# Narrower weight loads in four of six levels of a chunked linear attention

## The chip, the cores and the metric

The kernel runs on one core of one Trainium2 chip. Its time is the device time of one execution in microseconds. Below, TensorE is PE in the profile's rows, its weight loads are PEld, VectorE is DVE, ScalarE is ACT, GpSimd is POOL, and SyncE (which issues most DMAs) is SP.

## The reference, cut to what matters

The program is an attention with a decaying state, then a dense MLP, then a mixture of experts. Only the attention is touched by the change:

```
B, H, S, D = 2, 8, 768, 48
for t in range(S):
    cur = einsum('bhd,bhe->bhde', u * k[t], v[t])
    y[t] = einsum('bhd,bhde->bhe', r[t], state + cur)
    state = w[t][..., None] * state + einsum('bhd,bhe->bhde', k[t], v[t])
x = y.transpose(0, 2, 1, 3).reshape(1536, 384)
```

The MLP computes `relu(x @ w_in)**2 @ w_out` with 2048 hidden columns. The last part picks one of eight experts for each row and applies it.

## The kernel before, in words

**The attention in levels.** The 1536 rows are worked off in six pages of 256 rows (`NG = 6`, index `i`), and a page has two tiles of 128 rows (`t`). A row of a tile belongs to a chunk of 64 (`C = 64`, `h` is the chunk). Inside a chunk, the product of a query (`r`) with an earlier key (`k`) has to carry the decay between the two. The kernel builds this 64x64 matrix per head by doubling. At level `l` the chunk is cut into blocks of `2 * L` rows, with `L = 1 << l`. Keys of the left half of a block meet queries of its right half. TensorE multiplies (`level`, line 600 on), VectorE copies the entries that belong to the level into `AD` by a mask (`select`, line 1206), and VectorE then multiplies decays into keys and queries for the next level (`update`, lines 1192 and 1194). Level `l + 1` of a tile waits for that update (`upd`). There are six levels, 0 to 5.

**One level on TensorE.** The keys are the stationary operand (`x[rows, XW + c:XW + c + n]`, `n` columns), the right halves' 32 queries are the moving operand, and the result has `n` rows in PSUM. The loops over four head pairs, two chunks `h` and two heads `a` make 16 matrix products of 48 x n x 32 for a tile. `a` chooses partitions 0 or 64 for the operands, and `(h + a) % 2` chooses partitions 0 or 64 of PSUM, so four products in a row use the four 64x64 quarters of the array. A product in fp32 is two matmuls, each with its own weight load, in the trace: 32 loads for a tile and level, 64 for both tiles. `n` is `C`, 64, for levels 0 to 4, and 32 for level 5, where ScalarE copies one 32x32 block instead of the masked copy.

The masked copy at level `l` takes, of each pair of blocks, only the keys of the left half. The last left half ends at key `64 - L`. What lies in PSUM behind it isn't taken.

**The order.** Each engine has its own instruction list. A page's levels are not run in one piece. Page `i` is spread over the slots of page `i - 1`'s MLP, which has 16 slots: in a slot TensorE does the 9 matmuls of `hidden` (line 697), in some slots an attention step of both tiles, and the 6 matmuls of `project` (line 711). The table `LATER` puts a page's levels into slots -1, 1, 3, 5, 7 and 9, so two slots lie between two levels. Page 0 has no MLP beside it, and its levels run one behind the other. VectorE has, beside selects and updates, `square_low` (line 1254), one in every slot, and the router's dot products (line 1264). The weights of the dense MLP are loaded in 16 pieces through four staging buffers and split by ScalarE and VectorE (lines 964 and 1162) while pages 0 and 1 run. The fifth piece's load waits for `xl_ready[1]`, the end of page 0. After page 5 and its MLP come the experts, from about 307 us.

Of the kernel before, what the change touches and what calls it, by code (L numbers as in the profile page):

```python
# [5 lines left out]
def rwkv_moe_kernel(nc, cap, dims, krw, v, u, w_in, w_out, w_gate, w1, w2, gate_rows, out):  # L6
# [16 lines left out]
    C = 64  # L23
    NL = 6
    NMASK = 5
# [33 lines left out]
    with ctx:  # L59
# [200 lines left out]
        def need(eng, s, n):  # L260

            if not (isinstance(n, int) and n <= 0):
                eng.wait_ge(s, n)
# [311 lines left out]
        def _(pe):  # L575
# [5 lines left out]
            def right_of(x, c, l):  # L581

                return right_half(x[:, c:c + C], l)

            def half(h, a):

                return slice((h + a) % 2 * C, ((h + a) % 2 + 1) * C)
# [12 lines left out]
            def level(i, t, l):  # L600
                if l == 0:
                    pe.wait_ge(ld_kr[t][i % 2], 16 * (i // 2 + 1))
                    need(pe, xl_ready[t], i)
                else:
                    pe.wait_ge(upd[t], NL * i + l)
                    pe.wait_ge(sel[t], NMASK * i + l)
                if t == 0 and i >= 3 and l == NL - 1:
                    pe.wait_ge(rank_used, i - 2)
                x = KRW[t][i % 2]
                n = C if l < NMASK else C // 2  # L610
                for q in range(HP):
                    for h in range(2):
                        for a in range(2):
                            rows, c = slice(DP * a, DP * a + D), q * P + h * C
                            to = half(h, a).start
                            last = nc.tensor.matmul(pair[t][to:to + n, a, q * P:q * P + C // 2],  # L616
                                                    x[rows, XW + c:XW + c + n], right_of(x[rows, 0:XW], c, l),
                                                    start=q == 0, stop=q == HP - 1)
                if l > 0:
                    last.then_inc(att[t], 1)  # L620
# [152 lines left out]
            def attention(i, s, late):  # L773

                n, k = due(i, s)
                if n is None or late != (k == 0 or k > NL + 1):
                    return
                for t in range(1 if (n, k) == (1, 0) else 2):
                    if k < NL:
                        level(n, t, k)  # L780
                    if k == 0:
                        diagonal(n, t)
                    elif k == NL:
                        kk_rows(n, t)
                    elif k == NL + 2:
                        state_outputs(n, t)
                        if (n, t) == (0, 0):
                            unread(9)
                    elif k == NL + 3:
                        x_rows(n, t)  # L790
                        if (n, t) == (0, 1):
                            unread(5)
                if k == NL + 1:
                    outputs(n)

            def body(i, attn, mlp, gate):
                for s in range(NF):
                    if mlp:
                        hidden(i - 1, s)
                    if (i, s) == (1, 0):  # L800
                        level(1, 1, 0)
                        diagonal(1, 1)
# [745 lines left out]
```

## Time and profile before

| what | value |
|---|---|
| median of three runs | 462.81 us (460.69 to 464.67) |
| span of the profiled execution, from the first to the last instruction | 462.1 us |
| TensorE busy with matmuls | 441.2 us, 95% |
| TensorE busy with weight loads | 418.8 us, 91% |
| VectorE, ScalarE, GpSimd busy | 311.3, 251.2, 54.8 us |

No time is recorded for the profiled execution apart from its span; the span is 0.7 us below the median of the three runs. "Busy" is the time in which at least one instruction of the engine runs. A matmul's recorded duration has the way through the array in it, so 64 that run into one another are together far shorter than 64 durations. For the cost of a level the length of a merged row (64 loads, in us) tells more than the mean of one load.

### The profile page before, as it was taken

How to read it: one execution, taken by the hardware profiler on the slowest of the kernel's cores; microseconds unless marked ns; L12 is line 12 of the kernel's file. 1: busy time of each engine (PE TensorE's matmuls, PEld its weight loads, DVE VectorE, ACT ScalarE, POOL GpSimd, SP SyncE). 2: the span in 40 equal slices, each digit the busy share in tenths (PEclk: the TensorE clock that was granted, in tenths of full speed). 3: DMA queues.
4: the chain of work that ended last, by engine and by line, in shares of the span. 5: the costliest groups of instructions: out<-in, count | busy, mean ns of one | idle time of the engine just before them, and what ended most of it. 6: DMA issues, size and time to landing. Idle time of an engine off the chain costs nothing.

```text
span 462.1 us, 15274 instructions
## 1 busy us (share of the span) xinstructions
PE 441.2 (95%) x6266; PEld 418.8 (91%) x6266; DVE 311.3 (67%) x775; ACT 251.2 (54%) x515; POOL 54.8 (12%) x76
## 2 busy tenths in 40 slices
PE   4899999999999999999999999999999989999995
PEld 4788899999999999999999999998998879999994
DVE  4977966757786768677867746747565877678510
ACT  2253866356535654555454566565457876677421
POOL 8200000000000000001000100121020332221201
PEclk9999999999999999999999999999999999999999
DMA  8817795780130015001000139341866998620001
GB/s 280 276 47 237 264 321 180 256 343 4 50 144 1 3 41 188 1 3 38 2 3 3 38 146 333 81 168 37 293 204 222 302 362 260 220 64 1 32 0 43
DMA packets 35644, 63.44 MB, mean 137 GB/s; under 512 B 3980, under 2 KB 21950, under 8 KB 35568
## 3 DMA queue, kind: packets, MB, share of 16 engines
q1 hardware_dynamic: 33264, 57.88, 37.1%
q0 software_dynamic: 2304, 4.47, 2.6%
q8 instruction: 57, 0.93, 0.8%
q14 instruction: 19, 0.16, 0.1%
HBM read 50.77 MB, written 14.19 MB: 141 GB/s over the span
## 4 chain that ended last, share of the span: by engine, by line
PE 83%; DVE 7%; issue 4%; DMA 2%; ACT 2%; SPq 0%; POOLq 0%; DVEq 0%; ACTq 0%
PE bank L711 21%; PE bank L697 19%; PE pair L616 6%; PE bank L925 5%; PE bank L878 5%; PE pair L578 3%; PE pair L878 3%; PE pair L893 3%; PE bank L932 3%; PE bank L893 3%; DVE KRW L1192 2%; PE pair L637 2%; PE pair L672 2%; DVE AD L1213 2%; DMA stage<-in_moe_w_in 2%
## 5 line engine op out<-in xcount | busy, mean ns | idle before, releaser
L697 PE MATMUL bank<-XH,W 128*128 128x256 f32 x576 | 119.1, 283 | 0.2 <-ACT RB L1058 0.2
L711 PE MATMUL bank<-W,GH 128*128 128x384 f32 x372 | 98.9, 347 | 0.0
L697 PEld LDWEIGHTS bank<-XH,W 128*128 128x128 f32 x576 | 94.6, 188 | 1.2 <-issue 0.5
L697 PE MATMUL bank<-XL,W 128*128 128x256 f32 x288 | 80.5, 280 | 0.0
L1058 ACT ACTIVATE RB<-bank 128x256 f32<-128x256 f32 x96 | 36.7, 382 | 55.8 <-PE bank L697 55.2
L711 PEld LDWEIGHTS bank<-W,GH 128*128 128x128 f32 x372 | 62.0, 188 | 1.3
L711 PE MATMUL bank<-W,GL 128*128 128x384 f32 x186 | 62.7, 337 | 0.0
L1254 DVE TENSOR_TENSOR GL<-GG,GH 128x256 fp32r<-128x256 f32 x96 | 40.4, 421 | 29.5 <-ACT GH L964 27.3
L964 ACT ACTIVATE GH<-GG 128x256 fp32r<-128x256 f32 x96 | 40.1, 418 | 36.1 <-PE bank L711 34.1
L1192 DVE TENSOR_TENSOR KRW<-KRW 128x512 f32<-128x512 f32 x72 | 50.2, 698 | 6.9 <-PE pair L616 6.9
L616 PE MATMUL pair<-KRW 48*64 48x32 f32 (+1 forms) x2304 | 45.9, 228 | 8.9 <-DMA KRW<-in_krw 4.9
L616 PEld LDWEIGHTS pair<-KRW 48*64 48x64 f32 (+1 forms) x2304 | 40.3, 142 | 15.3 <-issue 6.1
L697 PEld LDWEIGHTS bank<-XL,W 128*128 128x128 f32 x288 | 54.1, 188 | 0.0
L1206 DVE COPY_PREDICATED AD<-mask,pair 128x256 f32<-128x256 uint32 x60 | 33.2, 553 | 23.1 <-PE pair L616 22.6
L1162 DVE TENSOR_TENSOR W<-raw,W 128x1536 fp32r<-128x1536 f32 x23 | 40.1, 1755 | 9.0 <-ACT W L964 9.0
L1064 ACT ACTIVATE GG<-RB 128x256 f32<-128x256 f32 x96 | 40.0, 417 | 5.5 <-DVE GL L1254 3.9
L925 PE MATMUL bank<-W,HH 128*128 128x384 f32 x192 | 39.0, 344 | 0.0
L711 PEld LDWEIGHTS bank<-W,GL 128*128 128x128 f32 x186 | 34.9, 187 | 0.0
L964 ACT ACTIVATE W<-raw 128x1536 fp32r<-128x1536 f32 x23 | 33.5, 1478 | 0.0
L549 POOL DMA_INDIRECT slots<-X,slot_u x8 | 8.3, 1038 | 212.3 <-DVE slot_u L1360 200.3
L1162 DVE TENSOR_TENSOR W<-stage,W 128x1536 fp32r<-128x1536 f32 x17 | 29.7, 1753 | 5.4 <-ACT W L964 5.4
L925 PEld LDWEIGHTS bank<-W,HH 128*128 128x128 f32 x192 | 33.3, 188 | 0.0
(163 smaller groups left out, 707.9 us busy)
## 6 DMA issues: line engine op xcount, KB each, us to landing
raw<-in_moe_w SPq DMA_DIRECT2D x23, 768.0 KB, 7.8
stage<-in_moe_w SPq DMA_DIRECT2D x9, 768.0 KB, 7.8
KRW<-in_krw SPq DMA_DIRECT2D x12, 512.0 KB, 6.0
slots<-X SPq DMA_DIRECT2D x8, 579.0 KB, 6.2
VV<-in_v SPq DMA_DIRECT2D x12, 288.0 KB, 7.0
KRW<-in_krw SPq DMA_DIRECT2D x12, 256.0 KB, 6.3
stage<-in_moe_w_in SPq DMA_DIRECT2D x4, 768.0 KB, 7.2
stage<-in_moe_w_out SPq DMA_DIRECT2D x4, 768.0 KB, 7.7
```

The source lines that it names most:

```text
L616: last = nc.tensor.matmul(pair[t][to:to + n, a, q * P:q * P + C // 2], x[rows, XW + c:XW + c + n], right_of(x[rows, 0:XW], c, l), start=q ...
L697: last = nc.tensor.matmul(bank[4 + f % 2][:, 0:2 * P], win[wa][:, c, f * P:(f + 1) * P], xa[:, c, :], start=n == 0, stop=n == 3 * KM - 1)
L711: last = nc.tensor.matmul(bank[6 + m][:, 0:DM], ga[(NF * g + f) % G3][:, cols], wout[wa][:, f, :], start=f == 0 and n == 0, stop=f == NF - ...
L878: last = nc.tensor.matmul(bank[HB[f % 3]][:, 0:2 * P], w1s(e, wa)[:, c, f * P:(f + 1) * P], xa[:, c, 0:2 * P], start=n == 0, stop=n == 3 * ...
L925: nc.tensor.matmul(y, HH[:, f, cols], w2s(e, wa)[:, f, :], start=f == 0 and wa == 0, stop=False)
L964: return nc.scalar.activation(dst, src, ACT.Copy)
L1058: nc.scalar.activation(RB[:, :], bank[4 + f % 2][:, 0:2 * P], ACT.Relu).then_inc(relu_ready, 1)
L1064: nc.scalar.activation(GG[f % 2][:, :], RB[:, :], ACT.Square).then_inc(g_ready, 1)
L1162: return tt(parts[1], src, parts[0].bitcast(F32), ALU.subtract).then_inc(wl_ready, 1)
L1192: last = tt(x, x, td.to_broadcast([P, 2, n, L]), ALU.mult)
L1206: nc.vector.copy_predicated(AD[t][:, :, :].rearrange("p x (g two j) -> p x g two j", two=2, j=L)[:, :, :, 1, :], m.to_broadcast([P, H, C / ...
L1254: tt(GL[k][:, :], GG[f % 2][:, :], GH[k][:, :].bitcast(F32), ALU.subtract).then_inc(gl_ready, 1)
```

## The change

At levels 1 to 4 the stationary operand gets only the keys up to the last left half: 64 - 2, 64 - 4, 64 - 8 and 64 - 16 columns. The product has as many rows in PSUM. Level 0 keeps 64 columns and level 5 keeps 32 (`64 - 32`, as before). The number of instructions, their order, their waits, the moving operand and where everything lies are unchanged.

```diff
@@ -607,7 +607,7 @@
                 if t == 0 and i >= 3 and l == NL - 1:
                     pe.wait_ge(rank_used, i - 2)
                 x = KRW[t][i % 2]
-                n = C if l < NMASK else C // 2
+                n = C - (1 << l) if l else C
                 for q in range(HP):
                     for h in range(2):
                         for a in range(2):
```

## Rows read from the trace of the kernel before

**Rows 1.** The page: busy time by engine, and the chain that ended last.

```profile
PE 441.2 (95%) x6266; PEld 418.8 (91%) x6266; DVE 311.3 (67%) x775; ACT 251.2 (54%) x515; POOL 54.8 (12%) x76
PE 83%; DVE 7%; issue 4%; DMA 2%; ACT 2%; SPq 0%; POOLq 0%; DVEq 0%; ACTq 0%
```

**Rows 2.** Stretches: from:to, length, PE busy (count), granted clock, DMA share, GB/s.

```profile
10.00:22.00 12.00, 9.64 (x328) 1.00 0.82 292
37.00:60.00 23.00, 21.91 (x434) 1.00 0.85 286
60.00:85.00 25.00, 25.00 (x520) 1.00 0.69 238
85.00:260.00 175.00, 174.22 (x3261) 1.00 0.19 68
```

**Rows 3.** Groups of weight loads by shape, 80 to 260 us: count, busy us, mean ns.

```profile
L616 PEld LDWEIGHTS pair<-KRW 48*64 48x64 f32 x1280 | 21.2, 134 | 4.4 <-DVE KRW L1194 1.2 <-issue 1.0
L616 PEld LDWEIGHTS pair<-KRW 48*32 48x32 f32 x256 | 2.6, 107 | 0.5
```

**Rows 4.** Instructions by time, page 2: a level of 64 columns, then level 5.

```profile
98.11 1.02 PEld L616 LDWEIGHTS pair<-KRW 48*64 48x64 f32 x64
...
109.07 0.65 PEld L616 LDWEIGHTS pair<-KRW 48*32 48x32 f32 x64
```

**Rows 5.** Instructions by time, page 1: 32 moving columns (L616), 64 moving (L595).

```profile
37.88 0.56 PEld L616 LDWEIGHTS pair<-KRW 48*64 48x64 f32 x32
...
38.34 0.56 PEld L595 LDWEIGHTS pair<-KRW,UK 48*64 48x64 f32 x32
```

**Rows 6.** Chain of waits, two steps of page 2: start, length, what.

```profile
98.18 1.06 PE pair L616 x64
99.25 1.25 PE bank L711 x6
100.49 1.06 PE bank L697 x9
101.55 1.06 PE bank L711 x6
102.61 1.05 PE bank L697 x9
103.66 1.06 PE pair L616 x64
```

**Rows 7.** VectorE and ScalarE around level 3 of page 2, by time; idle in brackets.

```profile
98.22 0.38 ACT L1058 ACTIVATE RB<-bank 128x256 f32<-128x256 f32 x1 [0.57 <-PE bank L697]
...
98.85 0.43 DVE L1206 COPY_PREDICATED AD<-mask,pair 128x256 f32<-128x256 uint32 x1 [2.11 <-PE pair L616]
```

**Rows 8.** Level 1 of page 2, by time: tile 1 waits for VectorE.

```profile
86.76 0.67 PE L616 MATMUL pair<-KRW 48*64 48x32 f32 x32
...
87.62 0.67 PE L616 MATMUL pair<-KRW 48*64 48x32 f32 x32 [0.19 <-DVE KRW L1194]
```

**Rows 9.** Page 0 by time: one tile's 32 loads, of 64 columns and of 32.

```profile
13.43 0.94 PEld L616 LDWEIGHTS pair<-KRW 48*64 48x64 f32 x32 [0.20 <-DVE KRW L1192]
...
21.41 0.51 PEld L616 LDWEIGHTS pair<-KRW 48*32 48x32 f32 x32 [0.70 <-DVE KRW L1192]
```

**Rows 10.** Chain of waits, page 0: a level, and what follows the last one.

```profile
16.97 1.12 PE pair L616 x32
...
18.45 0.70 DVE KRW L1192
...
19.19 1.12 PE pair L616 x32
...
24.72 0.73 issue
25.45 1.52 PE pair L637 x38
```

**Rows 11.** VectorE's idle time in page 0, by time.

```profile
18.11 0.43 DVE L1206 COPY_PREDICATED AD<-mask,pair 128x256 f32<-128x256 uint32 x1 [0.27 <-PE pair L616]
```

**Rows 12.** Chain of waits, page 1: a weight piece, then tile 1's level 3.

```profile
37.23 7.11 DMA stage<-in_moe_w_in
...
44.36 1.49 ACT W L964
...
51.25 0.67 PE pair L616 x32
...
56.33 1.06 PE pair L616 x64
```

## The prediction, made before the changed kernel had run

> **What bounds the kernel now.** I read the page first, for which engine the end hangs on. TensorE is busy 95% of the span and makes up 83% of the chain that ended last [rows 1]. A mean over the whole program doesn't say what a level is worth, so I cut it into stretches [rows 2]. From 60 to 260 us TensorE is idle for 0.8 us of 200: pages 2 to 5 are bound by it. In page 0 it is busy 9.6 of 12 us, and in page 1, 21.9 of 23. There something else has a part.
>
> Then the levels themselves. By shape, the 1280 loads of 64 columns between 80 and 260 us are 20 bursts of 64 and cover 21.2 us, 1.06 us a burst; the 256 of 32 columns are 4 bursts and cover 2.6 us, 0.65 us a burst [rows 3]. The rows by time say the same of single bursts, 1.02 and 0.65 us [rows 4]. Two things are to be seen. The mean load lasts 134 ns, yet 64 take 1.02 us, or 16 ns each, because four quarters of the array load side by side. And the burst gets shorter with fewer weight columns. That the moving side isn't the limit can be read too: 32 loads take 0.56 us with 32 moving columns behind each and the same 0.56 us with 64 [rows 5]. So a level's price is its weight loads, the thing which the change makes smaller.
>
> Last, whether a level lies on the path. In pages 2 to 5 the chain goes level, project, hidden, project, hidden, level, with nothing of another engine between [rows 6]. VectorE has waited 2.11 us when the level's first result comes, and ScalarE 0.57 us for its bank [rows 7]. Nobody is close to taking over from TensorE when it gets a tenth of a microsecond faster.
>
> **The change part by part.** Nothing is added or moved. What it removes is 2, 4, 8 and 16 weight columns at levels 1 to 4: 30 columns for each page, in each of a burst's 64 loads.
>
> *Price of a column.* The trace has 64 and 32 columns, nothing between.
> - The line through both is (1.02 - 0.65) / 32 = 0.0116 us for a column of one burst [rows 4]. This is the low end if the cost goes by columns, since a burst has fixed parts and the 32-column one may already stand on a floor of its own.
> - In proportion to 64 columns it would be 1.02 / 64 = 0.0159 us, the high end.
> - Page 0's loads run at about half the speed (0.94 us for one tile against 0.56 us in page 1), though the stretch's granted clock reads 1.00 [rows 2, 5, 9]. There one tile's 32 loads go from 0.94 to 0.51 us, (0.94 - 0.51) / 32 = 0.0134 us a column [rows 9].
> - If loads are priced by whole strips of 32 columns, it is zero: that is a rival.
>
> I take 0.0125 us for a burst of both tiles, nearer to the warm line, since it is the same state of the engine, and a little above it because of the likely floor at 32.
>
> The Trainium skill (TensorE: Matmul & The Clock Gate, "LDWEIGHTS (loading the stationary operand)") has a load take its column count over 1.2 in ns, whatever the number of rows. With four side by side that is an estimate of 16 / 1.2 ns, 0.0133 us, for a column of a burst, and 2.2 us for the sum below instead of 2.1. The two bursts of the trace differ by less, 0.0116 us a column; no row here is between 32 and 64.
>
> *Pages 2 to 5.* All four levels lie on the path, but for tile 0's half of level 1: tile 1 waits 0.19 us for VectorE behind it [rows 8], so what tile 0 saves there, half of 2 columns, only lengthens the wait. That leaves 29 columns: 4 x 29 x 0.0125 = 1.45 us (1.35 to 1.84).
>
> *Page 1.* Until about 51 us the chain runs through a weight piece's DMA, ScalarE's split and VectorE, and comes back to TensorE at tile 1's level 3 [rows 12]. Levels 1, 2 and tile 0's half of 3 are hidden behind that. Half of 8 columns and the 16 of level 4 count: 20 x 0.0125 = 0.25 us (0.23 to 0.32).
>
> *Page 0.* The chain alternates: a tile's 32 loads, 1.12 us, then VectorE's select and update, then the next level [rows 10]. VectorE idles 0.27 us in such a round [rows 11], so it can follow a level that is up to 0.27 us shorter. The largest cut, 16 columns, is 16 x 0.0134 = 0.21 us. All four fit: 30 x 0.0134 = 0.40 us. Behind it stands a gap of 0.73 us before the second tile's products, for which the chain names no releaser [rows 10]. If that is something with a date of its own, it eats the whole 0.40 us. I see no engine or transfer that would give it a date, and keep the 0.40 us, with 0 as the low end and 0.94 / 64 x 30 = 0.44 us as the high one. What is saved here isn't lost in page 1: the weight piece of the chain is issued at 37.23 us, after page 0's end released it [rows 12], and moves with it.
>
> *Sum.* 1.45 + 0.25 + 0.40 = 2.1 us; from both ends 1.6 to 2.6 us. The profiled span of 462.1 us would become 460.0 us. The span stands 0.7 us below the median of the runs shown; taken from the median, 462.81 - 2.1 = **460.7 us**, 0.45% less. What is late next where a stall goes: nothing in pages 2 to 5, and VectorE's round in page 0, which keeps 0.06 us of idle time at level 4.
>
> **The rivals.**
>
> *A: strips (no change).* A load of 33 to 64 columns may cost as one of 64. For it: the only two widths seen are one strip and two strips of 32, and both laws fit two points. Against it: nothing in the trace. Then levels 1 to 4 stay at 1.02 us and the median at 462.8 us. This is also the case in which the change doesn't do what it says. The Trainium skill bears on this (TensorE: Matmul & The Clock Gate, "Terms"): an instruction addresses the array by masks that select strips of 32 rows and 32 columns. By a price in such strips 62 to 48 columns are two of them, as 64 are, and the time is 462.8 us.
>
> *B: the saving is real and is lost elsewhere.* Page 0's gap eats 0.40 us, and in pages 2 to 5 VectorE takes over the pace at more places than the one row at level 1, as where it also has dot products. For it: that row exists in a page [rows 8]. Against it: VectorE's 2.11 us of idle time at a level [rows 7]. With half of pages 2 to 5 kept: 0.7 + 0.2 = 0.9 us, 461.9 us.
>
> *C: slower.* The four quarters stop overlapping. Now 64 loads take 1.02 us, 16 groups of four at 64 ns each with the ends shared out [rows 4], because a load for one quarter goes on while the others work. If a load narrower than the quarter counted as another division of the array, and the array emptied between such products, a group would cost about four times as much, a burst 3 x 1.02 = 3.1 us more. Of 4 levels in 5 pages (20 bursts) and page 0's four at half a burst and half speed (another 4) that is 24 x 3.1 = 73 us: 536 us. It decides from small amounts: 24 bursts need 0.19 us more each to reach 1%, or 12 ns for a group of four. For it: no row has an operand that doesn't fill its quarter or its strip. Against it: the 32-column loads, which fill half of such a quarter's width, run faster, and all products of a burst have the same width, so nothing changes inside one. A fixed price at a burst's edges would be small, since there the array already passes between 128 and 64 columns. The Trainium skill has the rule from which this would come (TensorEngine Tiling (Array Packing), "Key Properties"): changing the tiling mode, not just the tile, drains TensorE. No run here shows whether 62 columns count as another mode.
>
> **How the numbers follow.** The forecast gets 0.61, A 0.26, B 0.08, C 0.05. The three runs of the kernel before spread over 4 us, so a median can stand 1 us off on either side: about 1%, 4.6 us, is what a measurement of this kernel can tell from no change. The range takes the forecast's high end, 2.6 us, with 1 us of spread below, and A with 1 us above: **459.2 to 463.8 us**, which leaves out C and the tails. Forecast, A and B all lie within 1% (458.2 to 467.4 us). Slower by over 1% is C and a little for the runs' spread, 0.06. Faster by over 1% needs twice the sum and comes from the spread alone, 0.03. Within 1%: 0.91.
>
> **What would show it right or wrong.** The merged rows of levels 1 to 4 in page 2 should read 1.00, 0.97, 0.92 and 0.82 us where they read 1.02, and the chain's pieces shorten by the same. If all still read 1.02, it is A. If they shorten and the span doesn't, it is B: then look for a wait of TensorE on VectorE's line 1194 that grew beyond 0.19 us, and whether the gap at 24.7 us opened to over 0.73 us. A row above 1.02 us is C. In page 0 the step from one tile-1 level to the next, 2.22 us now, should shrink by 0.03 to 0.21 us. The forecast is also wrong if the price is not even in the columns, for instance steps of 8 or 16: then 62 and 60 columns read as 64 does, 56 and 48 are cheaper, and 0.4 us of the sum is missing.

## The result: 2.1 us less in the first comparison, 0.7 us in the second, within 1% in both

| | before | changed | ratio |
|---|---|---|---|
| median, first comparison | 461.46 us (20 runs) | 459.38 us (20 runs) | 0.9953, interval 0.9937 to 0.9970 |
| median, second comparison | 461.14 us (17 runs) | 460.41 us (12 runs) | 0.9988, interval 0.9970 to 1.0006 |
| span of the profiled execution | 462.1 us | 457.3 us | |

The forecast was 460.7 us, 2.1 us less than before. The first comparison says 2.1 us less in the medians, and the second, of which more below, 0.7 us. The two intervals touch only at the ratio 0.997, 1.4 us. The first median itself, 459.38 us, lies 1.3 us below the forecast and 0.2 us above the lower end of the range. The forecast stood on the median of three runs, 462.81 us, and twenty runs gave 461.46 us. The two profiled spans differ by 4.8 us. That is more than either comparison allows (at most 2.9 us), so a good part of it isn't the change.

The page of the changed kernel, its chain, and the same kinds of stretches as in [rows 1, 2] (columns: from:to, length, PE, PEld, DVE, ACT and POOL busy with counts, granted clock, DMA share, GB/s):

```profile
PE 437.4 (96%) x6266; PEld 415.2 (91%) x6266; DVE 311.3 (68%) x775; ACT 251.3 (55%) x515; POOL 56.4 (12%) x76
PE 85%; DVE 7%; issue 4%; ACT 2%; DMA 1%; POOLq 0%; SPq 0%; DVEq 0%; ACTq 0%
```

```profile
60.00:82.00 22.00, 22.00 (x441) 21.15 (x440) 13.62 (x28) 12.48 (x32) 0.00 (x0) 1.00 0.66 224
82.00:255.00 173.00, 172.18 (x3239) 165.58 (x3239) 129.43 (x406) 91.88 (x231) 6.53 (x6) 1.00 0.20 68
```

TensorE is still the bound: 0.8 us idle between 60 and 255 us, as before. The counts of instructions are the same. TensorE's busy time reads 3.8 us less, but a second profile of the kernel before reads 437.7 us, so most of that is not the change either.

The chain of waits through page 2 of the changed kernel (start, length, what), where before every level of 64 columns was a piece of 1.06 us [rows 6]:

```profile
89.84 1.01 PE pair L616 x64
90.86 1.24 PE bank L711 x6
...
95.27 0.96 PE pair L616 x64
...
100.64 0.85 PE pair L616 x64
...
105.91 0.69 PE pair L616 x50
```

These are levels 2, 3, 4 and 5, with 60, 56, 48 and 32 columns. Level 4 lost 0.21 us, level 3 0.10, level 2 0.05; the pieces between them kept their lengths, and level 5 its 0.69 us. So loads are paid by the column here, at (1.06 - 0.85) / 16 = 0.013 us for a column of a burst (the 64 loads of both tiles), and not by strips of 32.

Level 1 of page 2 in the changed kernel, by time, to be held against [rows 8]:

```profile
83.92 0.66 PE L616 MATMUL pair<-KRW 48*62 48x32 f32 x32
...
84.77 0.65 PE L616 MATMUL pair<-KRW 48*62 48x32 f32 x32 [0.20 <-DVE KRW L1194]
```

Tile 1 still waits for VectorE, 0.20 us where it was 0.19: what tile 0 saved went into the wait. And VectorE, by time, at level 3 of page 2, the row that answers to the second of [rows 7]:

```profile
95.88 0.43 DVE L1206 COPY_PREDICATED AD<-mask,pair 128x256 f32<-128x256 uint32 x1 [2.02 <-PE pair L616]
```

It waits 2.02 us for the result in place of 2.11. That is all the slack that was used up.

**Stretch by stretch.** The start times of a page's first level 1 and of its first products (line 637) cut both traces into stretches that hold the same instructions. The experts are counted from the first matmul of line 878, at 319.1 us in the kernel before. Two more profiles, of the same two kernels, are told below. All in us:

| stretch | before | before again | changed | changed again |
|---|---|---|---|---|
| start to page 0, level 1 | 10.17 | 10.11 | 9.73 | 9.85 |
| page 0: level 1 to products | 13.88 | 13.89 | 13.51 | 13.50 |
| to page 1, level 1 | 16.19 | 13.78 | 15.40 | 13.34 |
| page 1: level 1 to products | 27.50 | 26.89 | 26.25 | 26.59 |
| to page 2, level 1 | 19.03 | 19.03 | 19.03 | 19.03 |
| page 2: level 1 to products | 28.27 | 28.29 | 27.89 | 27.89 |
| page 3, same | 28.77 | 28.77 | 28.37 | 28.37 |
| page 4, same | 28.73 | 28.73 | 28.34 | 28.34 |
| page 5, same | 28.76 | 28.77 | 28.37 | 28.37 |
| page 5's products to the experts | 60.50 | 60.42 | 60.43 | 60.49 |
| experts to the end | 143.01 | 142.55 | 142.90 | 144.34 |

Pages 2 to 5 lost 0.38, 0.40, 0.39 and 0.39 us, 1.56 us in all, and page 0 lost 0.37 us. Those stretches repeat to 0.02 us from one profile to the next of the same kernel. The rest of the 4.8 us lies in stretches that don't repeat so well, page 1's among them.

### The profile page after: what moved, and what is told of

The parts are those of the page before. It is cut to its first block, busy times and chain, and to the rows that moved or that the text cites. A ratio compares the mean times of both kernels' runs of the same rounds, so it can differ in the third digit from the quotient of the medians.

```text
span 457.3 us, 15274 instructions
## 1 busy us (share of the span) xinstructions
PE 437.4 (96%) x6266; PEld 415.2 (91%) x6266; DVE 311.3 (68%) x775; ACT 251.3 (55%) x515; POOL 56.4 (12%) x76
## 4 chain that ended last, share of the span: by engine, by line
PE 85%; DVE 7%; issue 4%; ACT 2%; DMA 1%; POOLq 0%; SPq 0%; DVEq 0%; ACTq 0%
PE bank L711 22%; PE bank L697 20%; PE pair L616 6%; PE bank L925 6%; PE bank L878 5%; PE pair L578 3%; PE pair L878 3%; PE pair L893 3%; PE bank L932 3%; PE bank L893 3%; DVE KRW L1192 2%; DVE AD L1213 2%; PE pair L637 2%; PE pair L672 2%; PE pair L649 1%
## 5 line engine op out<-in xcount | busy, mean ns | idle before, releaser
L616 PE MATMUL pair<-KRW 48*64 48x32 f32 (+5 forms) x2304 | 43.2, 223 | 8.8 <-DMA KRW<-in_krw 4.9
L616 PEld LDWEIGHTS pair<-KRW 48*64 48x64 f32 (+5 forms) x2304 | 37.5, 138 | 15.5 <-issue 5.7
```

## The experiments

The timed ones are held against runs of the kernel before on the same chip. The first four share one set of 23 such runs (median 461.64 us), the two repeats of changed kernels at the end another of 17 (461.14 us), the repeat of the kernel before a third of 17 (461.54 us). The first theory: a column costs 0.0133 us in a burst of 64 loads, and what a burst loses, the program loses.

### One level alone

```diff
-                n = C if l < NMASK else C // 2
+                n = (C, C, C, C, 48, 32)[l]
```

> Only level 4 is narrowed, to 48 columns; levels 1 to 3 have 64 again. Theory (each weight column of a burst of 64 loads costs 0.0133 us, and what a burst loses the whole program loses): level 4's burst goes from 1.065 to 0.85 us to the next instruction, pages 1 to 5 give 5 x 0.213 us, page 0's tile 16 x 0.0133 = 0.21 us, together -1.3 us against the kernel before, ratio 0.9972. Rival (the price has steps, and the measured 2.1 us come from something else that the narrower loads set off, such as an earlier start of page 1's weight pieces): the level 4 burst is as short, but the time is either -2.1 us or not below the kernel before.

Ratio 0.9985 (0.9966 to 1.0004): 0.7 us less, in 12 runs. The interval, from 1.6 us less to 0.2 more, holds the theory's 1.3 us and no change too, but not the rival's 2.1 us. In its profile the stretches of pages 2 to 5 from level 1 to the products are 28.08, 28.54, 28.51 and 28.54 us, 0.19 to 0.23 below the kernel before, and page 0's is 13.67, 0.21 below. The groups of loads of this kernel, 78 to 255 us (count, busy us, mean ns):

```profile
L616 PEld LDWEIGHTS pair<-KRW 48*64 48x64 f32 x1024 | 17.1, 134 | 3.8 <-DVE KRW L1194 1.2 <-issue 1.0
L616 PEld LDWEIGHTS pair<-KRW 48*48 48x48 f32 x256 | 3.2, 121 | 0.5
```

The four bursts of 48 columns cover 0.8 us each, the sixteen of 64 columns 1.07 us. The level pays for itself alone in the stretches. The time is too coarse to show it.

### More columns in place of fewer

```diff
-                n = C if l < NMASK else C // 2
+                n = C
```

> The other direction: the kernel before with 64 columns at level 5 too, where it has 32. Theory: the burst of level 5 grows from 0.69 to 1.065 us (a floor keeps the 32-column burst from being 0.64), pages 1 to 5 pay 5 x 0.38 us, page 0's tile 0.43 us: +2.3 us against the kernel before, ratio 1.005. Rival (slack of the other engines takes up a change of this size): within 0.5 us of the kernel before.

Ratio 1.0063 (1.0039 to 1.0086): 2.9 us more, where 2.3 were expected and the interval gives 1.8 to 4.0. The stretches with level 5 grew: page 0's to 14.31 us (+0.43), those of pages 2 to 5 to 28.65, 29.11, 29.11 and 29.11 (+0.38, +0.34, +0.38, +0.35). The slack of the other engines took up nothing. The interval excludes no change, and the rival. In this profile the experts take 143.87 us, 0.86 us more than in the kernel before, and TensorE's granted clock reads 0.89 from 365 to 380 us; what that is comes below.

### The same price at another place

```diff
+                            n = D if i > 0 else DP
-                            last = nc.tensor.matmul(pair[t][DP * a:DP * (a + 1), h, c:c + D],
-                                                    KN[t][rows, q * P + DP * a:q * P + DP * (a + 1)], vv[rows, a, q, :],
+                            last = nc.tensor.matmul(pair[t][DP * a:DP * a + n, h, c:c + D],
+                                                    KN[t][rows, q * P + DP * a:q * P + DP * a + n], vv[rows, a, q, :],
```

> The changed kernel, and besides the state increments (line 649) load only the 48 columns of a head in place of 64 with 16 columns of padding, in pages 1 to 5; page 0 keeps 64. Theory: the same price at another place, in a burst of 64 loads with 48 moving columns: 16 x 0.0133 = 0.213 us for each of five pages, -1.07 us beside the change's -2.1: -3.2 us against the kernel before, ratio 0.993. Rival 1 (the moving side, 48 columns here in place of 32, sets this burst's pace): the burst stays at 1.04 us and the time is the changed kernel's. Rival 2 (ScalarE's copy of the increments and VectorE's state updates behind it set the end of this step): the burst shortens and the time doesn't.

Ratio 0.9949 (0.9931 to 0.9966), 2.4 us less, where 3.2 us were expected, which is at the very end of the interval (1.6 to 3.2). The bursts did what the price says. The increments' groups from 60 to 260 us, first of the changed kernel, then of this one:

```profile
L649 PEld LDWEIGHTS pair<-VV,UK 64*64 64x64 f32 x320 | 5.1, 135 | 0.0
```

```profile
L650 PEld LDWEIGHTS pair<-VV,UK 64*48 64x48 f32 x320 | 4.3, 122 | 0.0
```

Five bursts, 0.16 us less by this row; from the burst's first load to the next instruction on TensorE it is 0.87 in place of 1.08 us, 0.21. Rival 1 is out: 48 moving columns don't hold the burst at 1.04 us. From a page's products to the next page's level 1, where the increments lie, the stretch is 18.82 us where it was 19.03. Rival 2 is out too. But after the experts have begun, this profile lost 0.96 us against the changed kernel's (143.86 to 142.90 us); the cause is below.

### All four levels at 48

```diff
-                n = C - (1 << l) if l else C
+                n = (64, 48, 48, 48, 48, 32)[l]
```

> Levels 1, 2 and 3 have 48 columns like level 4; the products of keys 48 and up are left out there, so the output is not the reference's. Theory: 64 columns a page are gone in place of 30. Pages 2 to 5: 4 x 0.84 = 3.4 us, page 1 about 0.5 us (its levels 1 and 2 are hidden), page 0 four levels of 0.21 us, 0.8 us: -4.7 us against the kernel before, ratio 0.990. Rival (the other engines' slack is used up by the first tenth of a microsecond of a burst): levels 1 to 3 shorten, new waits on VectorE appear in front of the next level, and the time stays near the changed kernel's -2.1 us.

Ratio 0.9920 (0.9891 to 0.9949), 3.7 us less in 6 runs, with the expected 0.990 inside. The stretches of pages 2 to 5 are 27.55, 28.02, 27.98 and 28.01 us, 0.72 to 0.75 below the kernel before. I had written 0.84. I forgot there that tile 0's half of level 1, 0.11 us here, only lengthens tile 1's wait, and with it the sum fits. The waits of TensorE from 60 to 255 us:

```profile
PE pair L616 <- DVE KRW L1194: 1.2, 4, 0.3
```

The wait at level 1 grew from 0.2 to 0.3 us, four times, and no other appeared. In pages 2 to 5 even 0.21 us at every level is inside the slack of the other engines.

Not in page 0. Its stretch is 13.40 us, 0.48 below the kernel before, where I had written 0.8. The chain of waits at page 0's level 1, first of the kernel before, then of this one:

```profile
11.51 0.73 DVE KRW L1192
...
12.28 1.12 PE pair L616 x32
```

```profile
12.13 0.72 DVE AD L1206
12.85 0.53 DVE KRW L1192
```

TensorE's 1.12 us have left the chain, and VectorE's copy and update stand in their place. The copy takes 0.72 us here, where it takes 0.43 us later in the page [rows 11], and VectorE has no idle time in front of it. So level 1 has nothing to give in page 0. Counted from VectorE's masked copy at 10.95 us (10.97 before) to the products, the page lost 0.60 us, which is nearly the three cuts of 0.21 us at levels 2 to 4. The rest up to 0.48 is in the start of the stretch: tile 0's level 1 began 0.93 us ahead of the same copy and not 0.80, and nothing came of it. Of this page the rival was right at one level in four.

### Where a load stops getting cheaper

```diff
-                n = C - (1 << l) if l else C
+                n = (64, 44, 40, 36, 34, 32)[l]
```

> Widths 44, 40, 36 and 34 at levels 1 to 4, to find where a load stops getting cheaper; the products of the keys behind them are left out, so the output is not the reference's. Only the bursts are read, not the time. Theory: 0.0133 us a column goes on down to a floor that the 32-column burst (0.686 us to the next instruction, where 0.638 would be in line) already stands on: level 2 with 40 columns 0.745, level 3 with 36 columns 0.69, level 4 with 34 columns 0.69 us in place of 0.665. Rival (steps of 8 or 16 columns, which 60, 56 and 48 can't tell from a line with certainty): 44 and 40 as 48 (0.85 us), 36 and 34 as 40 or as 32.

Levels 2, 3 and 4 of page 2 of this kernel, by time:

```profile
92.08 0.70 PEld L616 LDWEIGHTS pair<-KRW 48*40 48x40 f32 x64
...
97.24 0.67 PEld L616 LDWEIGHTS pair<-KRW 48*36 48x36 f32 x64
...
102.37 0.65 PEld L616 LDWEIGHTS pair<-KRW 48*34 48x34 f32 x64
```

From first matmul to the next instruction that is 0.745, 0.709 and 0.693 us, and 0.686 with 32 columns. So 64, 60, 56, 48 and 40 columns lie on a line with 0.0133 us a column (1.065, 1.012, 0.958, 0.852, 0.745), with no steps of 8. At level 1, with 44 columns, tile 1's 32 loads take 0.465 us where 64 columns took 0.598, which is the same price. Below 40 it flattens: 0.009 us a column to 36, 0.008 to 34, 0.003 to 32. The floor I expected is there, softer than "0.69 from 36 on".

### What comes next: the moving side

```diff
+                            two = right_of(x[rows, 0:XW], c, l)
+                            if 0 < l < NMASK:
+                                two = bass.AP(two.tensor, two.offset, [two.ap[0], [-(1 << l), 2], *two.ap[1:]])
-                            last = nc.tensor.matmul(pair[t][to:to + n, a, q * P:q * P + C // 2],
-                                                    x[rows, XW + c:XW + c + n], right_of(x[rows, 0:XW], c, l),
+                            last = nc.tensor.matmul(pair[t][to:to + n, a, q * P:q * P + (C if 0 < l < NMASK else C // 2)],
+                                                    x[rows, XW + c:XW + c + n], two,
```

> The changed kernel with 64 moving columns in place of 32 at levels 1 to 4; the second 32 are the left halves of the queries, whose products nobody reads. It asks what comes next when the weight loads get cheaper. Theory: the 32-column floor comes from somewhere between loads and matmuls, and in the kernel before 32 loads take 0.56 us with 32 and with 64 moving columns, so at 64 columns the moving side is at most as long as the loads. [...] If the moving side is shorter, the bursts stay at 1.01, 0.96 and 0.85 us.

Levels 2, 3 and 4 of page 2, loads by time:

```profile
89.41 0.98 PEld L619 LDWEIGHTS pair<-KRW 48*60 48x60 f32 x64
...
94.87 0.98 PEld L619 LDWEIGHTS pair<-KRW 48*56 48x56 f32 x64
...
100.33 0.96 PEld L619 LDWEIGHTS pair<-KRW 48*48 48x48 f32 x64
```

The weights have 60, 56 and 48 columns and the burst no longer cares: 1.05, 1.05 and 1.04 us from first matmul to the next instruction. The bursts don't stay at 1.01, 0.96 and 0.85 us. Pages 2 to 5 take 28.26, 28.73, 28.71 and 28.74 us, at most 0.04 us less than in the kernel before. With 64 moving columns the moving side holds the burst, just under the price of 64 weight columns, 1.065 us. The second 32 columns are read by an access pattern with one step more; no run tells the width from the pattern. Taken as the width, the change gains because the level's moving operand is half as wide as its stationary one, and narrower loads at line 595, 64 by 64, would bring next to nothing. No run tried that.

### Page 0 alone

```diff
-                n = C if l < NMASK else C // 2
+                n = C - (1 << l) if l and (i == 0 or l == NL - 1) else C
```

> Only page 0 has the narrower loads; pages 1 to 5 are as in the kernel before. The stretch from page 0's level 1 of tile 0 to its first products is read (13.88 us in the kernel before, 13.51 us in the changed one), not the time. Theory: 13.5 us, since VectorE's idle 0.27 us a level lets it follow, and the gap of 0.73 us before tile 1's products stays as long. Rival (page 0's end has a date of its own): the levels are shorter and the gap grows by the same 0.4 us.

The stretch is 13.50 us, as the theory says. The chain of waits of this kernel in page 0:

```profile
14.82 1.07 PE pair L616 x32
...
16.99 1.02 PE pair L616 x32
...
19.11 0.91 PE pair L616 x32
...
23.83 0.61 PE pair L637 x16
24.48 1.43 PE pair L637 x42
```

Levels 2, 3 and 4 of tile 1 take 1.07, 1.02 and 0.91 us where each took 1.12 [rows 10]. The gap of 0.73 us in front of tile 1's products is 0.04 us here. It is 0.18 us in the kernel before's second profile and 0.72 us in the changed kernel's first: it comes and goes with and without the change. The theory had it as long as before, which was wrong, but the rival is out: the gap did not grow by what the levels lost. That page 0's 0.37 us reach the end of the program is not shown by this. The next stretch, to page 1's level 1, runs from 13.3 to 16.3 us over the profiles.

### Both kernels again

> The kernel before, once more, with a profile of its own. It asks what of the 4.8 us between the two profiled spans is chance. Theory: from page 1's products to the experts the stretches repeat to 0.1 us, while the stretch from page 0's products to page 1's level 1 (16.19 us in the first profile, 13.3 to 15.4 in those of the other kernels) comes out shorter, near 13.4 to 15 us, since it depends on when TensorE's clock rises. Rival (that stretch belongs to the kernel before, and the change has shortened it): again 16.2 us. Time: ratio 1 within its interval.

> The changed kernel once more, beside the narrower increments on the same chip. Theory: ratio 0.9953 to the kernel before, as the first time; in the profile levels 2 to 4 at 1.01, 0.96 and 0.85 us, whatever the first 40 us and the experts do. Rival (the first comparison was favoured by the chip): nearer to 1.

> The narrower increments once more. Up to the experts the first profile gained 0.21 us a page, as the price of a column says; its time was only 0.1 us below the changed kernel's first median, and its profile had TensorE's clock at the lower level for 3.4 us in the expert stage. Theory (that fall of the clock comes and goes): over both sets of runs about 1 us below the changed kernel, 0.9925. Rival (the shorter pages bring the fall about): again no more than 0.3 us below the changed kernel, with the fall in the profile again.

*The kernel before.* Ratio 0.9999 to itself (0.9978 to 1.0021, 12 runs), span 458.3 us: of the 4.8 us between the first two profiles, as much as 3.8 can be chance. Its stretch from page 0's products to page 1's level 1 was 13.78 us, not 16.19. Where most of that comes from can be seen at nine matmuls which only keep TensorE busy. First the kernel before, then the same kernel again, by time:

```profile
29.47 3.25 PE L685 MATMUL bank<-W 128*128 128x384 f32 x9
```

```profile
28.69 1.83 PE L685 MATMUL bank<-W 128*128 128x384 f32 x9 [0.87 <-issue]
```

The same nine take 3.25 or 1.83 us. The granted clock reads 1.00 in both, so that the early level isn't in its rows, but the durations are those of TensorE at half speed in the one and at full speed in the other. In the kernel before's first profile products, increments and all of these nine ran at half speed (eight of the nine last 522 ns each, against 334 to 338 ns in the second), in the second profile only a part of the products (the increments' matmuls last 303 ns on average in the first, 218 ns in the second).

*The changed kernel.* Ratio 0.9988 (0.9970 to 1.0006), nearer to 1, as the rival has it; the expected 0.9953 lies outside. Pages 0 and 2 to 5 repeat to the hundredth (table above), page 1 doesn't, and the experts don't: 144.34 us. Granted clock from 365 to 380 us (columns: stretch, length, PE busy, clock, DMA share, GB/s), of the changed kernel, then of it again:

```profile
365.00:380.00 15.00, 12.75 (x76) 1.00 0.98 335
```

```profile
365.00:380.00 15.00, 14.20 (x74) 0.89 0.84 283
```

And the chain at the same matmuls, in the same order:

```profile
366.52 2.30 PE pair L893 x9
368.82 2.05 PE bank L893 x9
```

```profile
365.31 3.05 PE pair L893 x9
368.36 2.90 PE bank L893 x9
```

A fall of the clock to the lower level, 1.2 GHz, for a part of the 15 us costs 0.75 + 0.85 = 1.6 us at these 18 matmuls. The first profile of the narrower increments has the same 0.89 there and 3.09 and 2.86 us at the same 18 matmuls, which more than covers its 0.96 us. Level 5 at 64 columns has it too. A mean clock of 0.994 or less over a run seems to mark such a fall: 8 of 32 runs of the changed kernel, and of the 69 of the kernel before whose clock is on record 10, of which 8 in one set of 17 and none in another. It isn't the change's doing as far as these counts can tell. It doesn't explain the second comparison: without its 4 such runs the median of the 12 is 460.27 us in place of 460.41, and without the first set's 4 it is 459.30 in place of 459.38. Why the second comparison gave 0.7 us stays open. Over all sets, on several chips, the medians are 461.49 us for the kernel before (89 runs) and 459.64 us for the changed one (32 runs), 1.9 us apart.

*The increments again.* Ratio 0.9927 (0.9902 to 0.9952), 3.4 us less. Without the fall of the clock in its profile, span 455.2 us, and the experts' stretch 142.89 us. The expected ratio 0.9925 is met, and the rival is out. The expected 1 us below the changed kernel isn't settled by the times: in the first sets the medians differ by 0.1 us, in the second, on one chip, by 3.0 us (457.38 to 460.41), and over both by 0.6 us (458.99 us in 17 runs, 459.64 in 32). The stretches give about 1.05 us, 0.21 us for each of five pages. By the medians it is the fastest of the kernels that compute the reference.

## Why the prediction was right

**The bound and the path.** TensorE bounds pages 2 to 5, and a level lies on the path whole. The chain, the stretches and both directions (level 5 wider, all four at 48) show it. Tile 0's half of level 1 is the exception, as forecast.

**The price of a column.** Taken at 0.0125 us for a burst, it is 0.0133. The line from 64 to 32 columns gave 0.0116 because 32 stands on a floor, as supposed; the proportional 0.0159 was too high. Page 0's 0.0134 us, for one tile at half speed, was the better guide to two tiles at full speed: at half speed 32 columns seem to stand clear of the floor. That 32 and 64 moving columns had taken the same 0.56 us [rows 5] was read rightly for 32, but it hid how near the moving side of 64 lies: 1.04 to 1.05 us against 1.065.

The Trainium skill (TensorE: Matmul & The Clock Gate, "LDWEIGHTS (loading the stationary operand)") has a load take its columns over 1.2 in ns, and with four loads side by side the estimate was the same 0.0133 us. The traces agree from 64 to 40 columns and not below.

**Pages 2 to 5.** 1.45 us predicted, 1.56 measured, all of the difference from the price: 4 x 29 x 0.0133 = 1.54.

**Page 0.** 0.40 predicted, 0.37 measured, and page 0 alone shows that it reaches the page's products. Levels 2 to 4 gave 0.05, 0.10 and 0.21. Level 1 gave nothing (a piece of 1.12 us, as before), and here the prediction's "all four fit" was wrong. It took VectorE's 0.27 us of idle time from a later round; at level 1 VectorE has none. The changed kernel's masked copy behind that level, by time, starts without an idle time in front of it:

```profile
12.98 0.74 DVE L1206 COPY_PREDICATED AD<-mask,pair 128x256 f32<-128x256 uint32 x1
```

This cost 0.03 us here, and about 0.2 us with 48 columns at every level.

**Page 1.** 0.25 us predicted. With 64 columns the stretch took 27.50, 26.89 and, in the kernel with page 0 alone narrowed, 26.65 us; in the two profiles of the changed kernel 26.25 and 26.59. Most of this spread is at level 3, by time, in the order page 0 alone, before again, changed, changed again:

```profile
47.12 1.14 PE L616 MATMUL pair<-KRW 48*64 48x32 f32 x64
```

```profile
47.46 1.40 PE L616 MATMUL pair<-KRW 48*64 48x32 f32 x64
```

```profile
48.26 1.03 PE L616 MATMUL pair<-KRW 48*56 48x32 f32 x64
```

```profile
46.32 1.36 PE L616 MATMUL pair<-KRW 48*56 48x32 f32 x64
```

In the second and fourth a wait is inside (in the kernel before's first profile the trace names VectorE's line 1194). The level behind it is clear of that: from the start of level 4 to that of level 5 it is 5.48 us in all three profiles with 64 columns and 5.27 us in both of the changed kernel. So 0.21 us of the term are shown. The two profiles without the wait differ by 0.40 us, the two with it by 0.30. So what the prediction had hidden, levels 1, 2 and half of 3, is hidden only in executions in which VectorE is late, and there in part. The term is 0.21 to 0.40 us.

**Sum.** 1.56 + 0.37 + 0.21 to 0.40 is 2.1 to 2.3 us, against 2.1 us forecast. The first comparison has it (1.4 to 2.9 us), the second (interval from 1.4 us less to 0.3 more) doesn't. That the first medians differ by just the forecast 2.1 us is in part luck, as the second comparison's 0.7 us shows. So is the time's place in the range: the starting point, 462.81 us, was 1.35 us above the median of twenty runs, and the measured 459.38 us is inside only by the 1 us left for the runs' spread. What bears the forecast out is the stretches.

**The rivals.** A (strips of 32) is refuted by every burst. B (lost elsewhere) is refuted in pages 2 to 5 by VectorE's wait that stayed at 0.20 us, and for the gap in page 0; VectorE took no more than page 0's level 1 and, in some executions, part of page 1. C (quarters no longer overlap) is refuted: a burst of 62 or 60 columns is no longer than one of 64. 62 columns are no other mode of the array, or changing to it costs nothing here.

**What I had not weighed** is that a single profile's span holds several microseconds of chance, in two places above all: the moment at which the clock rises in the first 35 us, and its fall among the experts.

## What to carry to other kernels

In these bursts of small fp32 matmuls on the quarters of the array, the wider of the two operands set the cost: 64 columns on either side gave 1.04 to 1.065 us. Trim the stationary operand by the column, as far as the moving operand is narrower, and expect little more below about 40 columns beside 32 moving ones. A saving of a few tenths of a microsecond is proved by stretches that hold the same instructions in both traces, from several profiles. Medians don't prove it: with a scatter of 4 us, two comparisons of 12 to 20 runs gave 2.1 and 0.7 us for the same change. And read an engine's slack in the round that the change shortens, not in a neighbouring one.

## What was not expected of the hardware

- Weight columns are paid evenly at 64, 60, 56, 48 and 40 (0.0133 us a column for a burst of 64 loads), and at 36, 34 and 32 the burst of 0.709, 0.693 and 0.686 us hardly shrinks.
- With 64 moving columns, 60, 56 and 48 weight columns cost 1.05, 1.05 and 1.04 us: the moving side of 64 lies 0.02 us below the stationary side of 64, 1.065 us.
- The same kernel's nine matmuls of line 685 took 3.25 us or 1.83 us, with a granted clock of 1.00 in both rows.
